# Attention steps in another order: transpose units paired by bank, the ends moved to the left mixture's bank

## The reference, cut to what matters

```python
def _attn_ref(q, k, v):                      # (4, 8, 576, 64) each
    scores = scale * np.matmul(q, k.transpose(0, 1, 3, 2))
    mask = block_i >= block_j                # blocks of 64 positions
    scores = np.where(mask, scores, -1000000000.0)
    scores = scores - np.max(scores, axis=-1, keepdims=True)
    attn = np.exp(scores)
    attn = attn / (np.sum(attn, axis=-1, keepdims=True) + 1e-09)
    return np.matmul(attn, v).astype(np.float32)
```

## Time and profile before

| what | value |
|---|---|
| median of 3 runs | 693.97 us (693.97 to 694.03) |
| the profiled execution: its own time | 693.8 us |
| its span in the profile | 692.1 us |
| PE busy | 673.5 us (97%) |
| PEld busy | 518.6 us (75%) |
| DVE busy | 434.8 us (63%) |
| ACT busy | 405.0 us (59%) |
| POOL busy | 165.8 us (24%) |
| chain that ended last | PE 87%, DVE 5%, DMA 2%, issue 2%, ACT 2% |

### The profile page before, as it was taken

The page is one execution under the profiler, slowest core; times in us unless marked ns, Lnnn a source line. Parts: engine busy times, 40 slices in busy tenths (PEclk is TensorE's granted clock), DMA queues, the critical chain, the costliest instruction groups (busy, mean ns, idle before and its releaser), DMA issues.

```text
span 692.1 us, 12915 instructions
## 1 busy us (share of the span) xinstructions
PE 673.5 (97%) x3982; PEld 518.6 (75%) x3982; DVE 434.8 (63%) x1049; ACT 405.0 (59%) x992; POOL 165.8 (24%) x228
## 2 busy tenths in 40 slices
PE   7999999999999999999999999999999999999996
PEld 4565556565689999898888898899889989864442
DVE  6666767676757676577657766676567656745222
ACT  5766666676865566556655666566656665542221
POOL 2676676767732000001000100020002000203111
PEclk9999999999999999999999999999999999999999
DMA  6655755553211001100010002000200010079171
GB/s 167 165 135 146 196 146 146 128 160 99 86 54 58 1 1 45 49 0 11 29 62 0 9 10 81 0 0 0 91 0 13 0 46 0 11 262 358 48 266 26
DMA packets 79470, 53.71 MB, mean 78 GB/s; under 512 B 61256, under 2 KB 64328, under 8 KB 79424
## 3 DMA queue, kind: packets, MB, share of 16 engines
q1 hardware_dynamic: 76048, 50.50, 24.5%
q0 software_dynamic: 1968, 1.86, 1.0%
q10 hardware_dynamic: 1408, 0.79, 0.4%
HBM read 41.18 MB, written 16.28 MB: 83 GB/s over the span
## 4 chain that ended last, share of the span: by engine, by line
PE 87%; DVE 5%; DMA 2%; issue 2%; ACT 2%; SPq 1%; ACTq 0%; DVEq 0%; POOLq 0%
PE hidden L1065 9%; PE hidden L1067 9%; PE hidden L1066 9%; PE rows_out L1078 9%; PE rows_out L1076 9%; PE rows_out L1077 9%; PE turned L389 8%; PE scores L356 6%; PE mixed L413 5%; PE scores L362 2%; PE hidden L1181 2%; PE rows_out L1196 2%; PE mixed L401 2%; DMA softplus_done<-x_sorted 1%; PE turned_y L1105 1%
## 5 line engine op out<-in xcount | busy, mean ns | idle before, releaser
L1289 ACT ACTIVATE mag<-hidden 128x384 f32<-128x384 f32 x96 | 47.1, 491 | 151.0 <-PE hidden L1067 149.2
L1065 PE MATMUL hidden<-x_parts,w_in_high 128*128 (+1 forms) x384 | 132.8, 346 | 0.6 <-DVEq L1482 0.6
L1067 PE MATMUL hidden<-x_parts,w_in_low 128*128 (+1 forms) x384 | 129.4, 337 | 0.0
L1066 PE MATMUL hidden<-x_parts,w_in_high 128*128 (+1 forms) x384 | 129.3, 337 | 0.0
L1015 POOL DMA_INDIRECT x_sorted<-y,slot x18 | 20.5, 1140 | 402.3 <-DVE slot L1531 398.7
L1078 PE MATMUL rows_out<-w_out_high,g_low 128*128 128x512 f32 x288 | 114.1, 396 | 0.0
L1076 PE MATMUL rows_out<-w_out_high,g_high 128*128 128x512 f32 x288 | 113.6, 395 | 0.4 <-DVE g_low L1489 0.4
L1077 PE MATMUL rows_out<-w_out_low,g_high 128*128 128x512 f32 x288 | 113.5, 394 | 0.0
L285 POOL TENSOR_SCALAR probs<-probs,inverse 128x128 f32<-128x128 f32 (+3 forms) x128 | 66.6, 539 | 62.3 <-DVE inverse L619 62.3
L1065 PEld LDWEIGHTS hidden<-x_parts,w_in_high 128*128 128x128 f32 x384 | 72.1, 188 | 8.5 <-issue 3.1
L1489 DVE TENSOR_TENSOR g_low<-g,g_high 128x384 fp32r<-128x384 f32 x96 | 54.8, 570 | 36.4 <-DVE g L1480 33.6
(11 more groups left out here) (200 smaller groups left out, 1057.0 us busy)
## 6 DMA issues: line engine op xcount, KB each, us to landing
whole_w<-in_moe_w_dram SPq DMA_DIRECT2D x12, 1024.0 KB, 9.5
x_heads<-x_pair SPq DMA_DIRECT2D x16, 288.0 KB, 2.1
x_raw<-x_heads SPq DMA_DIRECT2D x6, 768.0 KB, 5.6
out_dram<-y SPq DMA_DIRECT2D x6, 768.0 KB
v_nat<-in_v_dram SPq DMA_DIRECT2D x32, 128.0 KB, 2.4
stage<-in_moe_w_in_dram SPq DMA_DIRECT2D x8, 512.0 KB, 3.7
q_nat<-in_q_dram SPq DMA_DIRECT2D x30, 128.0 KB, 2.6
k_nat<-in_k_dram SPq DMA_DIRECT2D x30, 128.0 KB, 2.7
```

The lines of the kernel that those rows point to most:

```text
L1065: nc.tensor.matmul(o, win["high"][:, k, cols], high, start=(k == 0), stop=False)
L1066: nc.tensor.matmul(o, win["high"][:, k, cols], low, start=False, stop=False)
L1067: last = nc.tensor.matmul(o, win["low"][:, k, cols], high, start=False, stop=(k == K - 1))
```

## The change

For steps 2 to 14, PE's list becomes: scores 0 and 1; p0, p1; `mix_right(p-2)`; p2a, q; scores 2; p2b, p3a; scores 3; k, p3b; `mix_left(p-1)`; scores 4; ends; p4end; p4. ACT and DVE get lists of their own for these steps. The ends (from pair 2 on) and p4end leave the units: they go to columns 256 to 511 of `mixed[:, 0]`, with semaphores of their own, and DVE copies both at the end of its step. Copies by ACT and DVE out of that bank are kept apart by waits in `copy_left`, `copy_p4end` and `mix_left`. In step 0, ACT copies k of pair 1 (DVE did), and the early inverse comes ahead of the ends' copy. In step 1, ACT's copies of p0 and p2a come sooner. The diff, cut to its core:

```diff
-        UNITS = ("p0", "p1", "p2a", "q", "p2b", "p3a", "k", "p3b", "ends", "p4", "p4end")
+        UNITS = ("p0", "p1", "p2a", "q", "p2b", "p3a", "k", "p3b", "ends", "p4")
...
-                if step < PAIRS - 1 if name in ("q", "k", "ends") else step > 0:
-                    by = "copied_by_scalar" if name in BY_SCALAR or (step, name) == (-1, "k") else "copied_by_vector"
+                if step < (1 if name == "ends" else PAIRS - 1) if name in ("q", "k", "ends") else step > 0:
+                    by = "copied_by_scalar" if name in BY_SCALAR or name == "k" and step < 1 else "copied_by_vector"
...
+        ends_at = mixed[:, 0, SPLIT:SPLIT + P]
+        p4end_at = mixed[:, 0, SPLIT + P:SPLIT + 2 * P]
+        def ends_counted(p):
+            return min(p, PAIRS - 1) - 1
...
             def load_qk(p):
-                if p > 1:
+                if p in (2, 3):
                     sp.wait_ge(s["turned_ready"], turned_count(p - 3, "ends"))
+                if p > 3:
+                    sp.wait_ge(s["ends_turned"], ends_counted(p - 2))
...
+            def turn_ends(p):
+                pe.wait_ge(ends_loaded[p % 2], 32 * (p // 2 + 1))
+                if p < 2:
+                    bank_free(p - 1, "ends")
+                    to = bank(p - 1, "ends")
                 else:
+                    to = ends_at
...
+            def turn_p4end(p):
+                pe.wait_ge(s["probs_scaled"], 9 * p + 9)
+                nc.tensor.transpose(p4end_at[0:TAIL, :], probs_end[:, P * FULL:S], ident[:]).then_inc(s["p4end_turned"], 1)
...
-                elif i == (0 if p > 0 else FULL):
-                    pe.wait_ge(s["copied_by_vector"], copies[p - 1, "ends"][1])
+                elif p > 0 and i == 0:
+                    pe.wait_ge(s["copied_by_vector"], copies[p - 1, "k" if p > 1 else "q"][1])
+                    if p == 1:
+                        pe.wait_ge(s["copied_by_scalar"], copies[0, "k"][1])
+                elif i == FULL:
+                    if p < 2:
+                        pe.wait_ge(s["copied_by_vector"], copies[p - 1, "ends"][1])
+                    else:
+                        pe.wait_ge(s["ends_copied"], ends_counted(p))
...
                 need(pe, s["mixed_left_copied"], p)
+                need(pe, s["ends_copied"], ends_counted(p + 1))
+                need(pe, s["p4end_copied"], p)
...
+                if 1 < p < PAIRS - 1:
+                    turn_probs(p - 1, "p2a", 5, [(0, 2, c) for c in range(3)])
+                    turn_qk(p + 1, "q")
+                    score(p, 2)
+                    turn_probs(p - 1, "p2b", 6, [(1, 2, c) for c in range(3)])
+                    turn_probs(p - 1, "p3a", 7, [(0, 3, c) for c in range(4)])
+                    score(p, 3)
+                    turn_qk(p + 1, "k")
+                    turn_probs(p - 1, "p3b", 8, [(1, 3, c) for c in range(4)])
+                    mix_left(p - 1)
+                    score(p, 4)
+                    turn_ends(p + 1)
+                    turn_p4end(p - 1)
+                    turn_probs(p - 1, "p4", 9, [(0, 4, c) for c in range(4)])
+                    continue
...
-                if load:
-                    turn_qk(p + 1, "ends")
+                if p == 0:
+                    turn_ends(1)
                 score(p, 4)
+                if p == 1:
+                    turn_ends(2)
                 if turn:
+                    turn_p4end(p - 1)
                     turn_probs(p - 1, "p4", 9, [(0, 4, c) for c in range(4)])
-                    turn_probs(p - 1, "p4end", 9, [(0, 4, 4)])
...
             def copy_left(p):
                 act.wait_ge(s["mixed_left_ready"], p + 1)
+                need(act, s["ends_copied"], ends_counted(p + 2))
+                act.wait_ge(s["p4end_copied"], p + 1)
...
+                if p == 1:
+                    copy_probs(0, "p0", 0, (0, 1))
                 exponent(p, 0, 0)
                 exponent(p, 0, 1)
+                if 1 < p < PAIRS - 1:
+                    copy_probs(p - 1, "p0", 0, (0, 1))
+                    exponent(p, 1, 0)
+                    exponent(p, 1, 1)
+                    copy_probs(p - 1, "p2a", 2, (0,))
+                    copy_right(p - 2)
+                    copy_probs(p - 1, "p2b", 2, (1,))
+                    copy_probs(p - 1, "p3a", 3, (0,))
+                    exponent(p, 2, 0)
+                    exponent(p, 2, 1)
+                    exponent(p, 3, 0)
+                    exponent(p, 3, 1)
+                    copy_end(p - 1)
+                    exponent(p, 4, 0)
+                    continue
                 exponent(p, 1, 0)
-                if turn:
+                if p == 1:
+                    copy_probs(0, "p2a", 2, (0,))
+                if p > 1:
                     copy_probs(p - 1, "p0", 0, (0, 1))
                 exponent(p, 1, 1)
...
                 exponent(p, 2, 1)
+                if p == 0:
+                    act.wait_ge(s["turned_ready"], turned_count(0, "k"))
+                    nc.scalar.copy(kT[:, 1, 0:P * FULL], bank(0, "k")).then_inc(s["copied_by_scalar"], 1)
...
+            def copy_p4end(p):
+                need(dve, s["ends_turned"], ends_counted(p + 2))
+                dve.wait_ge(s["p4end_turned"], p + 1)
+                nc.vector.tensor_copy(probsT[0:TAIL, :, FULL, P * FULL:S],
+                                      p4end_at[0:TAIL, :].rearrange("p (a q) -> p a q", a=2)).then_inc(s["p4end_copied"], 1)
...
                     invert(p - 1, True)
                     copy_probs(p - 1, "p1")
+                if 1 < p < PAIRS - 1:
+                    copy_qk(p + 1, "q")
+                    maximum(p, 2)
+                    maximum(p, 3)
+                    copy_qk(p + 1, "k")
+                    invert(p, False)
+                    copy_probs(p - 1, "p3b")
+                    maximum(p, 4)
+                    copy_p4end(p - 1)
+                    copy_ends(p + 1)
+                    continue
...
                 maximum(p, 3)
-                if load:
+                if p == 0:
+                    invert(p, False)
+                if 0 < p < PAIRS - 1:
                     copy_qk(p + 1, "k")
...
-                if load:
-                    copy_qk(p + 1, "ends")
-                invert(p, False)
+                if p == 0:
+                    copy_ends(1)
+                if p > 0:
+                    invert(p, False)
                 maximum(p, 4)
                 if turn:
-                    copy_probs(p - 1, "p4end")
+                    copy_p4end(p - 1)
+                if p == 1:
+                    copy_ends(2)
```

More of the change, by code:

```diff
@@ L327, in turn_qk @@
                 to = bank(step, name)
[L328 to L332, removed]
-                else:
[L334 to L338, removed]
+                nat = q_nat if name == "q" else k_nat
+                for c in range(FULL):
+                    last = nc.tensor.transpose(to[:, c * P:(c + 1) * P],
+                                               nat[:, p % 2, c, :, :].rearrange("p a d -> p (a d)"), ident[:])
+                last.then_inc(s["turned_ready"], 1)
+            def turn_ends(p):
[3 more added lines that the diff above has]
+                    to = bank(p - 1, "ends")
+                else:
+                    to = ends_at
+                for n, nat in enumerate((q_nat, k_nat)):
+                    last = nc.tensor.transpose(to[:, n * TAIL:(n + 1) * TAIL],
+                                               nat[0:TAIL, p % 2, FULL, :, :].rearrange("p a d -> p (a d)"),
+                                               ident[0:TAIL, 0:TAIL])
+                last.then_inc(s["turned_ready" if p < 2 else "ends_turned"], 1)
+            def turn_p4end(p):
+                pe.wait_ge(s["probs_scaled"], 9 * p + 9)
+                nc.tensor.transpose(p4end_at[0:TAIL, :], probs_end[:, P * FULL:S], ident[:]).then_inc(s["p4end_turned"], 1)
             def score(p, i):
@@ L407, in mix_right @@
                 pe.wait_ge(s["copied_by_scalar"], copies[step, "p4"][1])
-                pe.wait_ge(s["copied_by_vector"], copies[step, "p4end"][1])
+                pe.wait_ge(s["copied_by_vector"], copies[step, "p3b"][1])
+                pe.wait_ge(s["p4end_copied"], p + 1)
                 need(pe, s["mixed_right_copied"], p)
@@ L428, in tensor @@
                 if p == 0:
-                    turn_qk(0, "ends")
+                    turn_ends(0)
                 if turn:
@@ L492, in exponent @@
                 if p > 0:
-                    if i < 2:
-                        name = ("p0", "p1")[i]
-                    else:
-                        name = (("p2a", "p2b"), ("p3a", "p3b"), ("p4end",))[i - 2][two]
-                    act.wait_ge(s["turned_ready"], turned_count(p, name))
+                    if i < FULL:
+                        name = (("p0", "p0"), ("p1", "p1"), ("p2a", "p2b"), ("p3a", "p3b"))[i][two]
+                        act.wait_ge(s["turned_ready"], turned_count(p, name))
+                    else:
```

(36 more changed lines are left out.)

7 lines of the change are left out of this document (4 added, 3 removed).

## The result

| what | before | after |
|---|---|---|
| median | 693.97 us (693.1 to 694.93, 5 runs) | 687.06 us (686.81 to 687.6, 5 runs) |
| ratio, 95% interval | | 0.9897, 0.9886 to 0.9908 |
| the profiled execution: its own time, its span | 693.8, 692.1 us | 686.81, 685.1 us |
| PE busy | 673.5 us (97%) | 670.5 us (98%) |
| DVE, ACT, POOL busy | 434.8, 405.0, 165.8 us | 432.5, 403.5, 166.4 us |

The kernel is 6.9 us faster, 1.0%; forecast were 6.7 us and 687.3. What has gone is time in which PE stood still, and the place of that can be read off. First the windows of the changed kernel, of one step and of what lies behind attention: PE is busy in all of the step's 11.48 us, where it was in 11.70 of 11.92.

What follows compares the result with a forecast made beforehand. PE was taken to bound the kernel, busy 11.70 of 11.92 us a step. 13 x 0.42 + 1.25 = 6.7 us off the profiled 693.8 gives 687.1, as median 687.3 us; 8-in-10 range 685.9 to 690.0.

Steps and rivals of the forecast that it cites:

- The bound and the place of the gain: PE bounds the kernel; within a step it stands still only before p2b, waiting for ACT's copy of p2a.
- the 0.42 us a step: Transposes p2a to p3b, steps 2 to 14: 3.27 us become 2.87 in runs of 7, 7 and 8; 0.42 saved.
- the signs: Traces expected if right: maskings 11.50 us apart, no ACT-copy bracket on PE, 7, 7, 8 transposes at 0.92, 0.92, 1.03.
- No wait comes back: In the new step each unit finds its bank copied in time; tightest is p3a, 0.35 us ahead.
- the layout: Predicted timetable of one new step, scores 0 at time 0 and end at 11.50 us, with the copies' times.
- Crossings: Switches between kinds of PE work: two go and two come per step, about 0.10 us each, so nothing taken.
- rival 3: Two crossings fewer per step, 13 x 0.2 = 2.6 us more gained, 684.7 us; chance 0.03.
- Rival 1: At the step's end p4 pays a new crossing after p4end, 0.10 us a step, 688.6 us; chance 0.13.
- rival 4: Slower: four weight shapes in a row at the step's end cost more crossings, about 695 us; chance 0.03 beyond 0.2%.
- rival 2: p3a waits for DVE's late copy of q, 0.2 us a step stays, 689.9 us; chance 0.12.
- The start: Steps 0 and 1: waits of scores 0, p1 and p2a shrink, 1.25 us saved, between 0.24 and 1.6.
- The sum: 13 x 0.42 + 1.25 = 6.7 us, with step 15 and the way out costing nothing.

Runs made afterwards that it cites:

- Experiment 1: Changed kernel with PE, ACT and DVE lists of steps 2 to 14 in the old order, new bank and changed start kept: 692.79 us.
- experiment 8: Kernel before, in steps 2 to 14 scores 2 moved behind q on PE and q's copy ahead of maximum 2 on DVE: 691.78 us.
- Experiment 7: Changed kernel with ACT's list of steps 2 to 14 as before, PE's and DVE's as changed: 698.6 us.
- experiment 2: Kernel before with the new order in steps 2 to 14; ends and p4end stay units of turned, ends ahead of scores 4: 694.69 us.
- experiment 5: Changed kernel with p4 ahead of p4end in steps 2 to 14: 687.57 us.
- experiment 9: Kernel of experiment 6, with SP loading q and k of pair 2 ahead of v of pair 1 and the first weights: 684.62 us.
- experiment 6: Changed kernel with the ends behind p4, next to scores 0 and 1 of the next step, in steps 2 to 14: 685.9 us.

## Why the prediction was right

**The bound and the place of the gain.** Right. PE's idle time ahead of p2b was the only one that the rows of a step show, and the 0.42 us a step were measured as 0.44 in most steps (11.917 to 11.475), 0.43 in the mean. Experiment 1 puts the old order back and the wait returns; experiment 8 takes it out by moving scores 2, with DVE's copy of q, and nothing else. Of the signs, the bracket is gone, and 7, 7 and 8 transposes take 0.91, 0.91 and 1.02 us.

**No wait comes back.** Right for this kernel, and the layout was good to 0.1 us in every place that I looked at. Experiment 7 shows that the layout could also have said no: one list in the old order, and the wait stands where the layout put it, with 0.85 us where I had 0.9. Yet in experiment 2 I made the very mistake that such a layout is there to prevent: I moved the ends and didn't ask which copy they wait for. The prediction had listed k's copy at 9.8, and the ends would have been due at 9.4.

**Crossings.** The same number as before, right: a step has five runs of transposes before and after (the title that rival 3 speaks of names no groups), and no step became shorter by the 0.2 us of rival 3. Taken as zero were the new neighbours, between -0.1 and +0.3 a step. Measured is next to nothing: p4 and p4end to the next scores 0.67 us and not 0.69, the ends 0.27 and not 0.26. Rival 1 is refuted by experiment 5, rival 4 by PE's rows of the step's end, where p4end starts 0.15 behind the last of the ends and p4 0.14 behind p4end; rival 2 by PE's rows, which have no bracket.

**The start.** This is the term that was mis-sized: 1.25 us foreseen, 0.86 measured, or 0.79 counted from step 0's own masking (6.87 to 23.85 against 6.94 to 24.71). The step that failed is "up to 0.8 us of that would lie in the wait before p2b". Timeline of PE in step 1 of the changed kernel:

```profile
15.11 0.55 PE L423 MATMUL turned<-ident,probs 128*128 128x128 f32 x3
16.39 0.66 PE L344 MATMUL turned<-ident,q_nat 128*128 128x128 f32 x4 [0.73 <-DMA q_nat<-in_q_dram]
16.88 0.49 PE L423 MATMUL turned<-ident,probs 128*128 128x128 f32 x3
```

The waits at which the prediction aimed did go: scores 0 of step 1 start at 12.24 (12.31 foreseen), and p2a at 15.11 (15.18). But q follows 1.28 us behind p2a, and p2b 1.77 and not 1.18: p2b's old wait doesn't hide the load. SP issues this load from 12.4 us on, before and after and in experiment 1, behind loads of v and of weights. How much it costs is shown by experiment 1, which has the same start, but whose step 0 happened to begin 0.92 us later (masking at 7.79), so that q had landed in time. Timeline of its PE in step 1:

```profile
16.01 0.55 PE L423 MATMUL turned<-ident,probs 128*128 128x128 f32 x3
16.61 0.63 PE L344 MATMUL turned<-ident,q_nat 128*128 128x128 f32 x4
```

Here q is 0.60 behind p2a without a bracket, and from the masking of step 0 to that of step 2 it takes 24.22 - 7.79 = 16.43 us, 1.34 less than before. Experiment 5 (24.52 - 8.08 = 16.44) and experiment 9, with the load sooner (16.45), agree. So the order of the start is worth 1.3 us, about what the prediction had for it, and the load takes 0.55 of it in the changed kernel. How much it takes differs from run to run: in experiment 7 q landed another 0.53 later, at 16.92.

**The sum.** 5.61 in the steps (5.46 foreseen), 0.86 at the start (1.25), 0.53 behind attention (0). Nothing suggests that the last is part of the change: over the eleven profiles (before, after, nine experiments) the stretch from step 15's masking to the end lies between 511.15 and 512.68 us, in no order that follows the edits. The smaller start (0.39 short) and this stretch (0.53 over) nearly cancel, and that is luck: the total fits better than its parts.

## What to carry to other kernels

Where two banks are filled in turn, the unit behind next must wait for a copy; look at each unit for what the engine does between that copy's source and it, and put work that needs none of these two banks (a product, a score) there. Units filled two by two between such works cost no more crossings than single ones, but every engine that copies must get its list changed with them: here PE's order with ACT's old list makes the kernel 4.2 us slower than before (698.6 against 694.38 in its series) instead of 6.9 faster. And a unit that can't be placed so may move to the unused columns of another bank, if its readers are kept apart by waits that have long been met.

## What the runs showed of the hardware

- Transposes and scores whose weights have the same shape, 64 by 128, follow each other without a crossing, and as each needs only 64 rows they start 0.01 us apart (experiment 6). Elsewhere one crossing more cost 0.12 us (experiment 8), and leaving transposes of 128 by 128 costs 0.10, to other transposes too (experiment 6). It is less between some shapes: 0.04 from the ends to p4end (0.15 against 0.11), 0.03 or nothing between transposes of 128 by 64 and 128 by 128 (experiment 5).
- PE starts 0.14 us after the end of the copy by ACT for which it waits (81.40 to 81.54 in experiment 7; 134.89 to 135.03 in experiment 8), and 0.15 after one by DVE (81.84 to 81.99 in experiment 2).
- What lies behind step 15's masking differs by up to 1.5 us between profiles of kernels that don't differ there, and the masking of step 0 comes at 6.87 to 8.43 us. Effects of less than 1 us are read from the stage's own rows, not from medians.
